# A pooled attention and two feed-forward layers in one kernel: the pooled rows of v are summed by TensorE instead of VectorE and DRAM

## The chip, the cores and the metric

The kernel runs on one core of one Trainium2 chip. The metric is device time in microseconds (us) of one execution, the median of several. Engines are named as the profile names them: PE is TensorE, DVE is VectorE, ACT is ScalarE, POOL is GpSimd, SP is SyncE, whose queue (SPq) issues nearly all transfers here.

## The reference

Attention over q, k, v of shape 4 batches x 8 heads x 576 positions x 64, in two parts that are added, followed by two feed-forward layers over 2304 tokens of width 512.

```python
q_d = q.reshape(B, H, Sd, factor, D).mean(axis=3)    # factor 4, Sd 144
k_d = k.reshape(B, H, Sd, factor, D).mean(axis=3)
v_d = v.reshape(B, H, Sd, factor, D).mean(axis=3)
out_d = sm_attn(q_d, k_d, v_d)                       # coarse: 144 x 144 a head
out_up = np.repeat(out_d, factor, axis=2)
mask = np.abs(pos[:, None] - pos[None, :]) < factor  # local: a band of 7
scores = np.where(mask, scale * q @ k.T, -1e9)
out_local = softmax(scores) @ v
x = out_up + out_local
# then rms norm, silu(x @ w_gate) * (x @ w_val) @ w_out, and relu(h)^2 layer
```

## The kernel before

**Coarse heads.** There are 32 of them (4 batches of 8), and PE takes them in 35 *slots*, `for n in range(HEADS + VAL_LAG)`. Slot n holds, in this order: 1 dummy matmul (3 in slots up to 8) that does nothing but keep PE running (L1845); the scores of head n (L1882); dummies again; the transposes of the exponentials of head n-2 (L1894); the value products of head n-3 (L1916); and, if `slot_units(n)` names one, a *unit*: the transposes that bring a third of one batch's pooled q or k into place (`turn_pooled`, L1864). Slots 5 to 10 hold the units of batch 1, slots 12 to 17 those of batch 2, slots 20 to 25 those of batch 3. For each head DVE takes the least score (`least`, L1567), ACT makes the exponentials (L1263) and copies the transposes out (`keep_turned`, L1255), and after each unit ACT copies it out of its PSUM bank CTR (`keep_pooled`).

**Rows of v for the coarse heads.** The four neighbouring rows of v have to be added. For batch 0 the rows come in two halves (`rawv0`, 72 partitions), and DVE adds them (`pool_v0`, L1544 and L1545) straight to `dv`, from which PE reads. For batches 1 to 3 `pool_v` (L1010, L1013) adds them on DVE in a layout of 128 partitions, ACT's queue stores the sum to DRAM (`store_vd`), and SP's queue loads it back in the layout of 72 partitions (`load_dv`). SP's queue is in order: `load_dv(1)` waits for that store, and all loads written behind it wait as well.

**Local part.** Tokens are cut into five tiles of 128 groups. POOL multiplies q and k windows (`qk_mult(a, n)`, 16 products a tile, L551) and probabilities and v windows (`pv_mult`, L565); DVE adds each product up (`qk_reduce` L596, `pv_reduce` L606); two product buffers tie the two together: product i waits until product i-2 was added up. Tile 0 holds its v windows in four places, so that heads 4 to 7 load only when a place comes free.

**Feed-forward.** After slot 34 PE runs 66 steps of gate, value and out matmuls (L782, L816 to L818): 18 for tile 0 (twelve of 256 columns, six of 512), then 12 for each further tile. Each weight piece is loaded, split in a high part (ACT, `weight_hi`) and a low part (`weight_lo`, mostly DVE). Tile 1's steps need tile 1's attention, made by POOL and DVE meanwhile. The order on each engine is written out by hand; DVE's has `hidden_mul(0)`, which waits for the first gate and value matmuls, ahead of `qk_reduce(1, 4)`. The second layer follows (L904 to L906, L922 to L924).

Of the kernel before, what the change touches and what calls it, by code (L numbers as in the profile page):

```python
# [44 lines left out]
UNIT0 = [("q", 0), ("k", 0), ("q", 1), ("k", 1), ("q", 2), ("k", 2)]  # L45
UNIT = [("q", 0), ("q", 1), ("k", 0), ("k", 1), ("q", 2), ("k", 2)]
UNITS = len(UNIT)
HEADS = B * H
# [7 lines left out]
UNIT_FROM = {1: 5, 2: 4, 3: 4}  # L56
# [14 lines left out]
PRODUCTS = [("qk", 0, n) for n in range(16)] + [("pv", 0, n) for n in range(16) if n not in ACT_PV[0]] + [("qk", 1, n) for n in range(16)]  # L71
# [75 lines left out]
def slot_units(n):  # L147

    for b in range(1, B):
        i = n - H * (b - 1) - UNIT_FROM[b]  # L150
        if 0 <= i < UNITS:
            return ((b, i),)
    return ()


def build(nc, q, k, v, w_gate, w_val, w_out, rms_g, w2_in, w2_out, s2, b2, out):
    y_scr = nc.dram_tensor("y_scr", [TILES, P, DT, W_], F32, kind="Internal").ap()
    c_scr = nc.dram_tensor("c_scr", [G, E], F32, kind="Internal").ap()
    v_scr = nc.dram_tensor("v_scr", [B, H * J, D], F32, kind="Internal").ap()

    with ExitStack() as ctx:
# [79 lines left out]
        rawv = [None] + [place(at, f"rawv{b}", [P, QT, FAC * D], F32) for b in (1, 3)]  # L241
        vs2 = place(at, "vs2", [P, 2, WIN * D], F32)
        assert at[0] <= att_start
        at = [wo_start]
        cs = place(at, "cs", [P, 4, 2 * J], F32)
# [5 lines left out]
        rawv = [None, rawv[1], place(at, "rawv2", [P, QT, FAC * D], F32), rawv[2]]  # L251
# [3 lines left out]
        kd = place(at, "kd", [P, 2, QT, D], F32)  # L255
        qd = place(at, "qd", [P, QT, D], F32)
        vd = place(at, "vd", [P, QT, D], F32)
# [47 lines left out]
        q0_pooled, k0_pooled, v0_pooled = sem("q0_pooled"), sem("k0_pooled"), sem("v0_pooled")  # L305
        rawv_loaded = [sem(f"rawv_loaded{b}") for b in range(B)]
        vd_stored, dv_loaded = sem("vd_stored"), [sem("dv_loaded0"), sem("dv_loaded1")]
        k_order, q_pooled = sem("k_order"), sem("q_pooled")
        k_pooled = [sem(f"k_pooled{b}") for b in range(B)]
        v_half, v_pooled = [sem(f"v_half{b}") for b in range(B)], [sem(f"v_pooled{b}") for b in range(B)]  # L310
# [9 lines left out]
        v_loaded = [sem(f"v_loaded{i}") for i in range(WSLOTS0)]  # L320
# [83 lines left out]
        def weight_hi(act, n):  # L404
# [5 lines left out]
            if n == FIRST_ORDER.index(("out", 0)):  # L410
                act.wait_ge(cpv, HEADS)
            if n >= NW1:
# [22 lines left out]
        def load_piece(sp, n):  # L435
            src, hi, lo, rows = piece(n)
            wait(sp, w_lo[n % SLOTS], n // SLOTS)
            if n == 0:
                sp.wait_ge(prod_ready, qk_at(0, 15) + 1)
# [55 lines left out]

        def q_win(a, h):
            n = slot_of(a, h)
            return qs[:, n, :] if n < 2 else qs2[:, n - 2, :]
# [5 lines left out]
        def v_win(a, h):  # L504
            n = slot_of(a, h)
            return vs[:, n, :] if n < 2 else vs2[:, n - 2, :]
# [13 lines left out]
        def load_v(sp, a, h):  # L520
            last = before_in_slot(a, h)
# [6 lines left out]
            load_window(sp, v, v_win(a, h), a, h, v_loaded[slot_of(a, h)], 48)  # L528
# [24 lines left out]
        def pv_mult(pool, a, n):  # L553
# [4 lines left out]
            if half == 0 or by_act(a, n - 1):  # L558
                pool.wait_ge(v_loaded[slot_of(a, h)], 48 * slot_turn(a, h))
# [7 lines left out]
        def pv_taps(act, a, n, f):  # L567

            h, half = divmod(n, 2)
            if f == 0:  # L570
                act.wait_ge(probs, a + 1)
                act.wait_ge(v_loaded[slot_of(a, h)], 48 * slot_turn(a, h))
# [413 lines left out]
        def store_vd(eng, b):  # L986
            eng.wait_ge(v_pooled[b], 1)
            eng.dma_start(v_scr[b].rearrange("(p t) d -> p t d", p=P), vd[:, :, :]).then_inc(vd_stored, 16)
# [990 lines left out]
```

## Time and profile before

| what | value |
|---|---|
| median of 3 runs | 980.24 us (979.86 to 981.27) |
| the profiled execution, its own time | 984.85 us |
| its span | 982.9 us |
| PE busy | 949.1 us, 97% |
| DVE busy | 537.4 us, 55% |
| ACT busy | 354.0 us, 36% |
| POOL busy | 368.4 us, 37% |

The profiled execution is 4.6 us above the median, and its span leaves out 1.95 us that lie around it. Engines overlap, so their busy times don't add up to the span. PE's busy time holds dummies, and it holds slow stretches too, in which PE was granted half of its clock; the windows below have the granted clock in their own column.

### The profile page before, as it was taken

The page shows a single profiled execution, that of the slowest core. Times are in us where ns is not written, and L with a number is a line of the kernel's source. Part 1 is how long each engine was busy: PE and PEld are TensorE (multiplying, and loading weights), DVE is VectorE, ACT ScalarE, POOL GpSimd, SP SyncE. Part 2 cuts the span into 40 slices and gives each one's busy share as a digit, 9 for nine tenths or more (in the row PEclk, how much of TensorE's full clock was granted, in tenths as well). Part 3 has the DMA queues.
Part 4 walks back from the last instruction along what each step waited for, and adds up shares of the span by engine and source line. Part 5 has one row for each costly group of instructions (what it writes and reads, how often), then busy time and mean ns, then how long its engine had stood idle before and what let it go on. Part 6 is the DMA issues. An engine that isn't in the chain of part 4 may idle for free.

```text
span 982.9 us, 13208 instructions
## 1 busy us (share of the span) xinstructions
PE 949.1 (97%) x5008; PEld 766.3 (78%) x5031; DVE 537.4 (55%) x813; ACT 354.0 (36%) x816; POOL 368.4 (37%) x192
## 2 busy tenths in 40 slices
PE   7888899989999999999999999999999999999998
PEld 4677699756777777777778998888888888888897
DVE  6888997886775765564542224444433443343343
ACT  2448854752324232422241444222322322222232
POOL 4757866777783876465600454000000000000000
PEclk9898799999999999999999999999999999999999
DMA  9898673433331331012003341102001100100010
GB/s 244 217 259 253 180 216 94 147 87 104 97 111 35 86 106 48 15 38 70 19 9 120 130 129 64 43 1 86 1 1 43 43 0 1 65 1 1 1 43 22
DMA packets 54379, 79.42 MB, mean 81 GB/s; under 512 B 9836, under 2 KB 37068, under 8 KB 52908
## 3 DMA queue, kind: packets, MB, share of 16 engines
q1 hardware_dynamic: 52284, 71.53, 24.8%
q10 hardware_dynamic: 2032, 7.05, 1.9%
q8 instruction: 40, 0.66, 0.3%
q14 instruction: 23, 0.19, 0.1%
HBM read 67.05 MB, written 11.50 MB: 80 GB/s over the span
## 4 chain that ended last, share of the span: by engine, by line
PE 78%; DVE 6%; DMA 4%; POOL 3%; ACT 3%; issue 2%; SPq 2%; ACTq 0%; DVEq 0%; POOLq 0%
PE bank L782 23%; PE bank L922 7%; PE bank L923 7%; PE bank L924 7%; PE bank L905 7%; PE bank L906 7%; PE bank L904 7%; PE bank L818 4%; PE bank L816 4%; PE bank L817 4%; POOL prod L551 3%; DMA rawv<-in_v_dram 2%; ACT prod_a L578 1%; DMA vs<-in_v_dram 1%; PE bank L726 1%
## 5 line engine op out<-in xcount | busy, mean ns | idle before, releaser
L551 POOL TENSOR_TENSOR prod<-qs,ks 128x896 f32<-128x896 f32 x80 | 177.7, 2244 | 89.7 <-DVE sc L596 62.9
L565 POOL TENSOR_TENSOR prod<-sc,vs 128x896 f32<-128x896 f32 x72 | 136.7, 2001 | 64.8 <-DVE x L606 32.7
L945 DVE SCALAR_TENSOR_TENSOR r<-bank,r 128x512 f32<-128x512 f32 (+1 forms) x80 | 51.1, 638 | 181.0 <-ACT r L933 181.0
L906 PE MATMUL bank<-y_h,w2i_l 128*128 128x512 f32 (+1 forms) x320 | 117.7, 368 | 0.0
L933 ACT ACTIVATE r<-bank 128x512 f32<-128x512 f32 (+1 forms) x80 | 44.4, 555 | 181.9 <-PE bank L906 181.2
L838 DVE TENSOR_TENSOR bank<-bank,u 128x512 f32<-128x512 f32 (+1 forms) x66 | 39.6, 599 | 118.0 <-PE bank L782 113.0
L782 PE MATMUL bank<-x_h,wv_h 128*128 128x512 f32 (+1 forms) x264 | 100.0, 390 | 0.0
L596 DVE TENSOR_REDUCE sc<-prod 128x14 f32<-128x896 f32 x80 | 85.7, 1078 | 18.0 <-POOL prod L551 18.0
L816 PE MATMUL bank<-h_h,wo_h 128*128 128x512 f32 (+1 forms) x264 | 93.1, 353 | 0.0
L818 PE MATMUL bank<-h_h,wo_l 128*128 128x512 f32 (+1 forms) x264 | 92.6, 351 | 0.0
L817 PE MATMUL bank<-h_l,wo_h 128*128 128x512 f32 (+1 forms) x264 | 92.5, 351 | 0.0
L782 PE MATMUL bank<-x_h,wg_h 128*128 128x512 f32 (+1 forms) x264 | 89.1, 359 | 1.0 <-ACT u L826 0.9
L782 PE MATMUL bank<-x_l,wv_h 128*128 128x512 f32 (+1 forms) x264 | 90.1, 353 | 0.0
L782 PE MATMUL bank<-x_l,wg_h 128*128 128x512 f32 (+1 forms) x264 | 88.2, 356 | 0.3 <-DVE x_l L759 0.3
L606 DVE TENSOR_REDUCE x<-prod 128x128 f32<-128x896 f32 x72 | 77.6, 1080 | 14.7 <-POOL prod L565 14.1
L922 PE MATMUL bank<-w2o_ha,g_h 128*128 128x512 f32 x216 | 84.3, 390 | 0.4 <-ACT y_st L852 0.4
L923 PE MATMUL bank<-w2o_la,g_h 128*128 128x512 f32 x216 | 84.2, 390 | 0.0
L924 PE MATMUL bank<-w2o_ha,g_l 128*128 128x512 f32 x216 | 84.0, 389 | 0.0
L939 ACT ACTIVATE g_h<-r 128x512 fp32r<-128x512 f32 (+1 forms) x80 | 47.1, 589 | 101.1 <-DVE r L947 101.1
L826 ACT ACTIVATE u<-bank 128x512 f32<-128x512 f32 (+1 forms) x66 | 34.2, 518 | 128.6 <-PE bank L782 128.5
L953 DVE TENSOR_TENSOR g_l<-r,g_h 128x512 fp32r<-128x512 f32 (+1 forms) x80 | 51.2, 639 | 52.5 <-ACT g_h L939 52.5
L832 ACT ACTIVATE h_h<-bank 128x512 fp32r<-128x512 f32 (+1 forms) x66 | 34.3, 519 | 110.1 <-DVE bank L838 110.1
(142 smaller groups left out, 1935.7 us busy)
## 6 DMA issues: line engine op xcount, KB each, us to landing
raww<-in_moe_w_out_dram SPq DMA_DIRECT2D x14, 512.0 KB, 4.1
ks<-in_k_dram SPq DMA_DIRECT2D x16, 280.0 KB
vs<-in_v_dram SPq DMA_DIRECT2D x16, 280.0 KB, 5.0
y_scr<-y_st ACTq DMA_DIRECT2D x4, 1024.0 KB, 5.7
raww<-in_moe_w_in_dram SPq DMA_DIRECT2D x8, 512.0 KB, 3.5
y_raw<-y_scr SPq DMA_DIRECT2D x4, 1024.0 KB, 4.8
out_dram<-o_st SPq DMA_DIRECT2D x16, 256.0 KB, 2.8
rawq<-in_q_dram SPq DMA_DIRECT2D x3, 1152.0 KB, 15.2
```

The source lines that it names most:

```text
L551: pool.tensor_tensor(dst, qv, kv, ALU.mult).then_inc(prod_ready, 1)
L565: pool.tensor_tensor(dst, pv, vv, ALU.mult).then_inc(prod_ready, 1)
L596: dve.tensor_reduce(sc[:, a % 2, n * 2 * BAND:(n + 1) * 2 * BAND], prod[:, at_ % 2, :].rearrange("p (s d) -> p s d", d=D), op=ALU.add, axi ...
L606: dve.tensor_reduce(x[:, 2 * half:2 * half + 2, h * D:(h + 1) * D], over(prod[:, at_ % 2, :], [[BAND * D, 2], [BAND, D], [1, BAND]]), op=A ...
L782: last = pe.matmul(o[:, 0:w], wt[:, m, kk, :], xs[:, kk, cols], start=i == 0, stop=i == 3 * DT - 1)
L816: pe.matmul(o, wo_h[:, m, cols], h_h[:, s % 3, 0:w], start=m == 0 and p != 1, stop=False)
L817: pe.matmul(o, wo_h[:, m, cols], h_l[:, s % 3, 0:w], start=False, stop=False)
L818: last = pe.matmul(o, wo_l[:, m, cols], h_h[:, s % 3, 0:w], start=False, stop=m == M1 - 1)
L906: last = pe.matmul(o, w2i_l[:, m, kk, :], y_h[t % 2][:, kk, 0:w], start=False, stop=kk == DT - 1)
L922: pe.matmul(o, g_h[:, r % 3, cols], wh[:, mh, :], start=m == 0, stop=False)
L923: pe.matmul(o, g_h[:, r % 3, cols], wl[:, mh, :], start=False, stop=False)
L924: last = pe.matmul(o, g_l[:, r % 3, cols], wh[:, mh, :], start=False, stop=m == M2 - 1)
```

## The change

The four rows of v are added by PE: four matmuls whose stationary operand is the identity, 72x72, and whose moving operand is rows of v, 72x512, in float32, accumulate in the bank CTR; ACT copies the result to `dv`. These are two more units a batch, ("v", 0) and ("v", 1). `pool_v0`, `pool_v`, `store_vd`, `load_dv` and the DRAM scratch go. Rows of v of all batches load in halves of 72 partitions, and each later half waits until PE has read the half before it in its buffer. Units now stand in slots 2 and 3 (the two v units of batch 0), 4 to 11, 12 to 19 and 20 to 27. Tile 0 gets eight places for v windows. The first two products of tile 1 move ahead of tile 0's pv products on POOL, `weight_lo(1)` moves behind `least(30)` on DVE.

```diff
-UNIT = [("q", 0), ("q", 1), ("k", 0), ("k", 1), ("q", 2), ("k", 2)]
+UNIT = [("q", 0), ("q", 1), ("k", 0), ("k", 1), ("v", 0), ("q", 2), ("k", 2), ("v", 1)]
+QK0 = 6
-UNIT_FROM = {1: 5, 2: 4, 3: 4}
+UNIT_FROM = 4
...
+    if n in (2, 3):
+        return ((0, QK0 + n - 2),)
+    b, i = divmod(n - UNIT_FROM, UNITS)
+    return ((b + 1, i),) if 0 <= b < B - 1 else ()
...
             if n < SLOTS:
-                eng.wait_ge(v_pooled[1], 1)
-                eng.wait_ge(v_pooled[3], 1)
+                eng.wait_ge(ctr_ps, UNITS * B)
...
-        def load_dv(eng, b):
-            eng.wait_ge(vd_stored, 16 * b)
-            wait(eng, cpv, H * (b - 1))
-            eng.dma_start(dv[0:JH, b % 2, :, :], v_scr[b].rearrange("(n p) d -> p n d", p=JH)).then_inc(dv_loaded[b % 2], 16)
...
-            load_rawv0(0)
+            load_rawv(0, 0)
+            load_qk(sp, 0, 1)
             load_rawq(1)
-            load_qk(sp, 0, 1)
+            load_rawv(0, 1)
             load_qk(sp, 0, 2)
-            load_rawv0(1)
...
+                if b > 1:
+                    sp.wait_ge(ctr_ps, UNITS * (b - 1) + UNIT.index(("v", g)) + 1)
+                sp.dma_start(rawv[1 + g][0:JH, :, :], rows).then_inc(rawv_loaded[g], 16)
...
+                if kind == "v":
+                    wait(act, cpv, H * (b - 1))
+                    act.activation(dv[0:JH, b % 2, H * g:H * (g + 1), :], CTR[0:JH, :].rearrange("p (h d) -> p h d", d=D), ACT.Copy).then_inc(ctr_evac, 1)
...
+                if kind == "v":
+                    if b == 0:
+                        pe.wait_ge(rawv0_loaded[g], 16)
+                    else:
+                        pe.wait_ge(rawv_loaded[g], 16 * b)
+                    pe.wait_ge(ctr_evac, n)
+                    rows = rawv0[0:JH, H * g:H * (g + 1), :] if b == 0 else rawv[1 + g][0:JH, :, :]
+                    for f in range(FAC):
+                        last = pe.matmul(CTR[0:JH, :], ident[0:JH, 0:JH], rows[:, :, f * D:(f + 1) * D], start=f == 0, stop=f == FAC - 1)
```

On PE, slots 2 to 4 of the kernel before, from the transposes of head 0 on (L1845 dummies, L1882 scores, L1894 transposes, L1916 value products, L1864 a unit of q):

```order
L1894 MATMUL bank<-ident,cs 72x72 x4
L1845 MATMUL bank<-ident 128x512 x3
L1882 MATMUL bank<-kT,qT 72x144 x2
L1845 MATMUL bank<-ident 128x512 x3
L1894 MATMUL bank<-ident,cs 72x72 x4
L1916 MATMUL bank<-dv,cpT 72x64 x4
L1845 MATMUL bank<-ident 128x512 x3
L1882 MATMUL bank<-kT,qT 72x144 x2
L1845 MATMUL bank<-ident 128x512 x3
L1894 MATMUL bank<-ident,cs 72x72 x4
L1916 MATMUL bank<-dv,cpT 72x64 x4
```

The same place of the changed kernel (its line numbers are its own: L1836 dummies, L1884 scores, L1896 transposes, L1917 value products, L1852 the new v units):

```order
L1896 MATMUL bank<-ident,cs 72x72 x4
L1852 MATMUL bank<-rawv_104,ident 72x512 x4
L1836 MATMUL bank<-ident 128x512 x3
L1884 MATMUL bank<-kT,qT 72x144 x2
L1836 MATMUL bank<-ident 128x512 x3
L1896 MATMUL bank<-ident,cs 72x72 x4
L1917 MATMUL bank<-dv,cpT 72x64 x4
L1852 MATMUL bank<-rawv_104,ident 72x512 x4
L1836 MATMUL bank<-ident 128x512 x3
L1884 MATMUL bank<-kT,qT 72x144 x2
L1836 MATMUL bank<-ident 128x512 x3
```

The scores of head 4 now stand behind both v units of batch 0, the second of which waits for the second half of batch 0's rows (`rawv0_loaded1`).

On SP's queue, the loads behind the last q and k windows of tile 0, before (L1036 rows of v of batch 2, L475 v windows, L1025 rows of q of batch 3, L994 `load_dv(2)`):

```order
L1036 DMA rawv_103<-in_v_dram 128x2304
L475 DMA vs<-in_v_dram 16x448
L475 DMA vs<-in_v_dram 15x192
L475 DMA vs<-in_v_dram 112x640
...
L1025 DMA rawq_106<-in_q_dram 128x9x256
L994 DMA dv<-v_scr 72x16x64
```

and in the changed kernel (L1030 the two halves of batch 2, L474 v windows, L528 the q window of tile 1's head 0):

```order
L1030 DMA rawv_94<-in_v_dram 72x8x256
L1030 DMA rawv_95<-in_v_dram 72x8x256
L474 DMA vs<-in_v_dram 16x448
L474 DMA vs<-in_v_dram 15x192
L474 DMA vs<-in_v_dram 112x640
...
L528 DMA qs<-in_q_dram 16x256
```

The wait for a store to DRAM has gone from the queue; in its stead the two halves wait for PE's units in slots 8 and 11, and all loads behind them with them.

## Rows read from the trace of the kernel before

**Rows 1.** Windows by stage: us, then busy us (x instructions), granted PE clock, DMA share, GB/s

```profile
13.50:38.80 25.30, 20.16 (x158) 14.33 (x155) 17.96 (x22) 9.98 (x42) 14.31 (x7) 1.00 1.06 242
38.80:71.80 33.00, 28.56 (x237) 24.03 (x237) 27.20 (x36) 13.65 (x54) 20.10 (x10) 0.86 0.88 247
71.80:122.70 50.90, 43.49 (x331) 36.66 (x329) 47.42 (x80) 43.15 (x160) 40.12 (x19) 0.77 0.70 208
122.70:209.00 86.30, 86.09 (x582) 74.92 (x585) 74.53 (x89) 51.63 (x129) 62.27 (x29) 0.97 0.51 150
209.00:231.00 22.00, 17.05 (x71) 11.27 (x71) 14.38 (x33) 10.24 (x17) 12.67 (x6) 0.92 0.22 63
231.00:983.00 752.00, 745.48 (x3601) 601.00 (x3620) 346.51 (x545) 221.84 (x408) 211.06 (x103) 1.00 0.15 49
```

**Rows 2.** Timeline of PE, slot 13: start, us, what

```profile
55.44 0.38 PE L1845 MATMUL bank<-ident 128*128 128x512 bf16 x1
55.65 0.66 PE L1882 MATMUL bank<-kT,qT 72*72 72x144 f32 x4
56.14 0.38 PE L1845 MATMUL bank<-ident 128*128 128x512 bf16 x1
56.36 0.41 PE L1894 MATMUL bank<-ident,cs 72*72 72x72 f32 x4
56.61 0.68 PE L1916 MATMUL bank<-dv,cpT 72*72 72x64 f32 x8
57.13 0.82 PE L1864 MATMUL bank<-ident,rawq 128*64 128x128 f32 x6
57.78 0.38 PE L1845 MATMUL bank<-ident 128*128 128x512 bf16 x1
```

**Rows 3.** Timeline of PE: where slots 4, 8 and 18 begin

```profile
20.52 0.81 PE L1845 MATMUL bank<-ident 128*128 128x512 bf16 x3
...
38.11 0.89 PE L1845 MATMUL bank<-ident 128*128 128x512 bf16 x3
...
71.38 0.63 PE L1845 MATMUL bank<-ident 128*128 128x512 bf16 x1
```

**Rows 4.** Timeline of PE: first transposes of x, first gate matmuls

```profile
115.38 1.94 PE L726 MATMUL bank<-ident,x 128*128 128x128 f32 x8 [1.38 <-ACT x L707]
...
122.69 1.20 PE L782 MATMUL bank<-x_h,wg_h 128*128 128x256 f32 x4
```

**Rows 5.** Instructions on rawv: duration ns min/median/max, first and last start

```profile
L1010 DVE TENSOR_TENSOR rawv<-rawv x3: 1343/1360/2649, 41.5 to 92.1; 128x1152 f32<-128x1152 f32 x3
L1013 DVE TENSOR_TENSOR vd<-rawv x3: 757/2141/2619, 42.9 to 93.5; 128x576 f32<-128x576 f32 x3
...
L1544 DVE TENSOR_TENSOR rawv<-rawv x2: 1211/2174/3137, 17.9 to 30.5; 72x1024 f32<-72x1024 f32 x2
L1545 DVE TENSOR_TENSOR dv<-rawv x2: 687/688/689, 19.1 to 33.7; 72x512 f32<-72x512 f32 x2
```

**Rows 6.** Waits of SP's queue to 125 us: us in total, times, longest

```profile
SPq L994 <- DMA v_scr<-vd: 34.8, 3, 15.5
```

**Rows 7.** Timeline of DVE: the second half of batch 0's v arrives

```profile
30.52 3.14 DVE L1544 TENSOR_TENSOR rawv<-rawv 72x1024 f32<-72x1024 f32 x1 [0.53 <-DMA rawv<-in_v_dram]
```

**Rows 8.** The page's groups of instructions: busy us, mean ns | idle before

```profile
L596 DVE TENSOR_REDUCE sc<-prod 128x14 f32<-128x896 f32 x80 | 85.7, 1078 | 18.0 <-POOL prod L551 18.0
...
L832 ACT ACTIVATE h_h<-bank 128x512 fp32r<-128x512 f32 (+1 forms) x66 | 34.3, 519 | 110.1 <-DVE bank L838 110.1
```

**Rows 9.** Windows after PE had sat idle: columns as in rows 1

```profile
37.40:44.00 6.60, 6.57 (x35) 4.90 (x36) 4.82 (x5) 1.61 (x6) 5.15 (x3) 0.60 1.02 244
...
68.90:82.80 13.90, 13.51 (x75) 11.15 (x76) 12.26 (x22) 9.72 (x42) 7.96 (x4) 0.52 0.70 207
...
110.00:127.00 17.00, 15.43 (x92) 13.68 (x93) 16.49 (x36) 13.53 (x33) 12.40 (x5) 0.51 0.45 135
```

**Rows 10.** Timeline of POOL: products of tile 1 after the first gate matmuls

```profile
130.51 11.31 POOL L551 TENSOR_TENSOR prod<-qs,ks 128x896 f32<-128x896 f32 x4 [5.64 <-DVE sc L596]
```

More of the change, by code:

```diff
@@ L69 @@
 ACT_PV = {0: (2, 6, 10, 13), 1: (2, 6, 10, 13)}
-PRODUCTS = [("qk", 0, n) for n in range(16)] + [("pv", 0, n) for n in range(16) if n not in ACT_PV[0]] + [("qk", 1, n) for n in range(16)]
+PRODUCTS = [("qk", 0, n) for n in range(16)] + [("qk", 1, 0), ("qk", 1, 1)]
+PRODUCTS += [("pv", 0, n) for n in range(16) if n not in ACT_PV[0]] + [("qk", 1, n) for n in range(2, 16)]
 EARLY = {2: 2, 3: 4, 4: 4}
@@ L240, in build @@
         at = [gl_start]
-        rawv = [None] + [place(at, f"rawv{b}", [P, QT, FAC * D], F32) for b in (1, 3)]
+        rawv = [None] + [place(at, f"rawv{g}", [P, H, FAC * D], F32) for g in range(2)]
+        at = [gl_start + 2 * QT * FAC * D * 4]
         vs2 = place(at, "vs2", [P, 2, WIN * D], F32)
@@ L244, in build @@
         at = [wo_start]
+        vs3 = place(at, "vs3", [P, H - WSLOTS0, WIN * D], F32)
         cs = place(at, "cs", [P, 4, 2 * J], F32)
@@ L319, in build @@
         qk_loaded = [sem(f"qk_loaded{i}") for i in range(WSLOTS0)]
-        v_loaded = [sem(f"v_loaded{i}") for i in range(WSLOTS0)]
+        v_loaded = [sem(f"v_loaded{h}") for h in range(H)]
         prod_ready, prod_used = sem("prod_ready"), sem("prod_used")
@@ L494, in before_in_slot, with v_turn, v_before @@
             return (0, h + WSLOTS0) if a == 1 else (a - 1, h + H - 2)
+        def v_turn(a, h):
+            return 1 if a == 0 else 1 + (H // 2) * (a - 1) + h // 2 + 1
+        def v_before(a, h):
+            if a == 0:
+                return None
+            if h >= 2:
+                return (a, h - 2)
+            return (0, h) if a == 1 else (a - 1, h + H - 2)
         def q_win(a, h):
@@ L504, in v_win @@
         def v_win(a, h):
-            n = slot_of(a, h)
-            return vs[:, n, :] if n < 2 else vs2[:, n - 2, :]
+            n = h if a == 0 else h % 2
+            return vs[:, n, :] if n < 2 else vs2[:, n - 2, :] if n < WSLOTS0 else vs3[:, n - WSLOTS0, :]
         def load_qk(sp, a, h):
@@ L520, in load_v @@
         def load_v(sp, a, h):
-            last = before_in_slot(a, h)
+            last = v_before(a, h)
             if last is not None:
@@ L1144, in _ @@
             pool.memset(ident[:, :], 0.0).then_inc(consts_made, 1)
-            for s_ in (ks, vs, ks2, vs2):
+            for s_ in (ks, vs, ks2, vs2, vs3):
                 last = pool.memset(s_[0:1, :, 0:(FAC - 1) * D], 0.0)
@@ L1265, in exponents @@
                                    accum_out=csum[0:JH, b % 2, 2 * h + a, 0:1]).then_inc(cexp, 1)
-            for i in range(UNITS):
+            for i in range(QK0):
                 keep_pooled(0, i)
@@ L1615, in _ @@
             least(15)
-            pool_v(dve, 2)
             least(16)
@@ L1622, in _ @@
             least(17)
+            qk_reduce(dve, 1, 0)
             softmax_norm(dve, 0)
+            qk_reduce(dve, 1, 1)
             pool_q(3)
@@ L1660, in _ @@
             add_pooled0(dve, 1)
-            weight_lo(dve, 1)
             least(29)
@@ L1664, in _ @@
             least(30)
-            qk_reduce(dve, 1, 0)
+            weight_lo(dve, 1)
             exponent_sums(3, 0)
@@ L1668, in _ @@
             least(31)
-            qk_reduce(dve, 1, 1)
             exponent_sums(3, 1)
@@ L1865, in turn_pooled @@
                     else:
-                        last = pe.transpose(to, qd[:, 3 * g + t, :] if kind == "q" else kd[:, 0, 3 * g + t, :], ident[:, :])
+                        last = pe.transpose(to, qd[:, 3 * g + t, :] if kind == "q" else kd[:, 3 * g + t, :], ident[:, :])
                 last.then_inc(ctr_ps, 1)
-            for i in range(UNITS):
+            for i in range(QK0):
                 turn_pooled(0, i)
                 if i % 2:
-                    keep_running(CSC[0], 3 if i < UNITS - 1 else 2)
+                    keep_running(CSC[0], 3 if i < QK0 - 1 else 2)
             for n in range(HEADS + VAL_LAG):
@@ L1905, in _ @@
                     pe.wait_ge(cpt_evac, g + 1)
[L1906 to L1909 removed]
+                    if h % 4 == 0:
+                        pe.wait_ge(ctr_evac, UNITS * b + (UNIT if b else UNIT0).index(("v", h // 4)) + 1)
+                    if h == 0:
                         wait(pe, co_ready, 2 * b - 1)
```

133 lines of the change are left out of this document (55 added, 78 removed).

## The prediction

> **What bounds the kernel now.** I read the windows by stage first [rows 1]. From 231 us on PE is busy 745.5 of 752 us at full clock: nothing in the change touches this part, so the kernel ends when it does because of the time at which this part begins. From 122.7 to 209 us PE is busy 86.1 of 86.3 us, with the steps of tile 0. Between them, 209 to 231 us, PE sits idle for 5.0 us and is granted 0.92 of its clock: it waits there for tile 1's attention. So two things can move the end: the time at which the coarse heads let PE go (122.69 us, the first gate matmul [rows 4]), and the time at which tile 1 is ready.
>
> The change works in the stretch before 122.7 us. There, from 13.5 us on, PE is busy 92.2 of 109.2 us, DVE 92.6, ACT 66.8, POOL 74.5 (the sums of the first three of rows 1). No engine is full; DVE and PE are nearest, and PE lost about as much by its clock (granted 0.86 and 0.77 in the second and third, 4.6 + 11.7 us) as it sat idle (17.0 us). SP's queue stood 34.8 us behind the trips through DRAM [rows 6].
>
> How full PE really is, one slot tells [rows 2]. Slot 13, with one dummy at a time and a unit of q, begins at 55.44 us and the next at 57.78: 2.34 us with no gap in it. Its parts, from start to start: a dummy 0.21, scores 0.49, a dummy 0.22, transposes 0.25, value products 0.52, the unit 0.65.
>
> **What goes.** On DVE ten additions: L1010 5.35 us in all, L1013 5.52, L1544 4.35, L1545 1.37 [rows 5], together 16.6 us. ACT loses three issues of stores. SP's queue loses the 34.8 us, but not for free, see below.
>
> **What comes on PE.** The trace has no float32 matmul of 512 columns that isn't rounded. The nearest row is the scores: two matmuls of 144 columns appear as four records and take 0.49 us [rows 2], 0.85 ns a column and record. At two records a matmul, 512 columns take 0.87 us, a unit of four 3.48 us, and the eight units 27.9 us at full clock, twice that at half. Bound below: one record a column, 13.9 us; above, the value products (eight records of 64 columns in 0.52 us, 1.02 ns) give 33 us. I take 27.9, because the scores are the same kind of instruction with the longer moving operand. A slot with a v unit then takes 2.34 - 0.65 + 3.48 = 5.17 us, one with no unit 1.69.
>
> The Trainium skill, in TensorE: Matmul & The Clock Gate, section Back-to-back issue gap, gives N / 2.4 GHz plus 2.5 ns a matmul, 0.216 us for 512 columns, and that would make 6.9 us of the eight units instead of 27.9. The trace disagrees for this type: by that rule two scores would take 0.13 us, and they take 0.49 [rows 2].
>
> **On ACT** eight copies of 72x512. The nearest row is `hidden_hi`, 519 ns [rows 8]: 4.2 us. ACT is busy 66.8 of 109.2 us and each copy stands behind the exponentials of its slot, so I cost it at nothing; if ACT is the one that holds a slot up (slots 19 to 27, where it also makes products of tile 0), it costs up to 0.5 us each, 1.6 us for the three units there. The new memset of vs3 and the loads of tile 0's last v windows are hidden: their products come tens of us later.
>
> **Slot by slot.** Before, slot 4 begins at 20.52 us [rows 3]. The first v unit puts 3.5 us ahead of that: 24.0. The second half of batch 0's rows arrived at 30.5 us [rows 7], which only DVE had to wait for, and PE worked on with slots 4 to 6. Now PE itself waits for it at the end of slot 3, with every later slot queued behind, and DVE, ACT and POOL behind PE's scores. One set of q and k windows (408 KB) fewer stands ahead of it: 1.7 us at 242 GB/s [rows 1]. So it lands at 28.8 us, PE sits idle 4.8 us, and slot 4 begins at 28.8 + 3.5 = 32.3.
>
> Slots 4 to 7 have six dummies each: 2.34 + 4 x 0.22 = 3.22 us, 12.9 together. Pooled k of batch 1 is made by DVE behind `least(6)` and a reduction (1.08 us [rows 8]), then 1.34 us of its own (same shape as L1010 [rows 5]); the reduction and the addition, 2.4 us, run while PE does 1 us of slot 6: I add 1.4. Slot 8 begins at 46.6, where it began at 38.11 [rows 3]: 8.5 us late.
>
> The clock: after an idle stretch PE was granted 0.60 for 6.6 us, or 0.52 for 13.9 us [rows 9], which lost 2.6 or 6.7 us. The new idle of 4.8 us will do one of the two; nothing excludes that it costs none. I take 2.6, the nearer in place, so slot 8 begins 11.1 us late.
>
> Slots 8 to 17 at full clock: slot 8 has six dummies and a v unit, 6.05; slots 11 and 16 5.17 each; the other seven 2.34 each; 32.8 us. Before they took 71.38 - 38.11 = 33.3 us [rows 3], with idle and slow stretches. So slot 18 begins 10.6 us late, and the unit time is paid for by idle time that PE had anyway.
>
> Slots 18 to 30 and the part of slot 31 ahead of x's transposes: three slots with v (19, 24, 27), seven with q or k (18, 20 to 23, 25, 26), three empty, and 1.2 us: 15.5 + 16.4 + 5.1 + 1.2 = 38.2 us. Before it was 115.38 - 71.38 = 44.0 us [rows 3, 4], a good part of it at 0.52 of the clock [rows 9] and behind ACT and DVE. With DVE 3.5 us lighter here and PE fuller, I take 2 us of idle: 40.2, so 3.8 us are given back. The transposes of x start 6.8 us late. DVE's chain for tile 0 does not come earlier: its last reduction stands behind `least(28)`, and that behind PE's slot 28.
>
> From the transposes to the first gate 7.3 us [rows 4], kept. The gate starts 6.8 us late.
>
> **After the gate.** POOL waits 5.64 us for `qk_reduce(1, 4)` [rows 10]. In DVE's order this stands behind `hidden_mul(0)`, and that behind PE's first value matmuls. So tile 1's chain moves with PE's gate; that POOL has two of tile 1's products behind it already only lengthens this wait. `weight_lo(1)`, moved behind `least(30)`, holds back piece 5 on SP's queue and two windows of tile 1 behind it, to about the time of that wait: nothing more. The idle time at 209 us stays as it is, since both its sides moved alike. For small slack on DVE I take off 0.3 us.
>
> **The sum.** 3.5 (first unit) + 4.8 (wait) + 3.5 (second unit) + the longer slots 4 to 7, so that slot 8 is 8.5 late; + 2.6 (clock) - 0.5 - 3.8 - 0.3 = +6.5 us. Against the profiled execution: its span goes from 982.9 to 989.4 us, its own time from 984.85 to 991.4. That execution lies 4.6 us above the median, so the median goes from 980.24 to 986.7 us.
>
> The skill also has a rule that speaks for the change: SBUF — State Buffer, section SBUF: two separate sides, says that a DVE operation with two SBUF inputs and a GpSimd operation lock each other out of a shared port pair. The trace agrees: the same addition took 757 and 2619 ns [rows 5]. By it POOL gains too, at most the 16.6 us of these additions, but POOL's products stand behind DVE's reductions and those behind PE's scores.
>
> **The rivals.**
> *DVE's relief and the free queue win (faster).* For it: DVE busy 47.4 of 50.9 us, and 34.8 us of SP's wait. The point from which it decides: the second half of v lands by 24.0 us and PE never drops its clock. Then slot 8 is 3.7 late, slot 18 3.2, the transposes 3.2 + 38.2 - 44.0 = 2.6 early, and the stretch of 17 us at 0.51 [rows 9] runs at full clock, of which I count 2.4 more. 980.2 - 5 = 975.2. Against it: loads were full all the while (DMA share 1.06 [rows 1]).
> *The delay is swallowed (no change).* PE has 5.0 us idle at 209 to 231 us and slow clock there [rows 1]: about 6.5 us. If tile 1 did not depend on the gate, that would hold 6.5 us of delay: 980.2. Against it stands the order on DVE.
> *PE stays at half clock (much slower).* A second drop like that of 13.9 us, 6.7 us [rows 9]: 993.4.
> *The units are cheap.* By the row of bf16 dummies (0.21 us for 512 columns [rows 2]) the eight cost 6.9 us. The wait for the second half stays, but slot 8 is then 5.9 late, slots 8 to 17 take 25.0 us and 18 to 31 30.4: whatever else binds then is DVE, with 16.6 us less; 976.
> The skill's rule on the issue gap, above, is this last rival.
> That the change doesn't do what it says, also partly holds: SP's queue trades the wait for DRAM for waits on PE's slots 8, 11, 16 and 19. That is in the forecast, since windows still arrive in time.
>
> **How the numbers follow.** Forecast 0.56, relief wins 0.17, swallowed 0.12, half clock 0.12, cheap units 0.03. The forecast's own bounds: clock cost 0 instead of 2.6, idle in slots 18 to 31 0 instead of 2, 982; clock cost 6.7 and idle 5, 994. The range 979 to 994.5 leaves out most of the two faster rivals, and little above. Within 0.2% (about 2 us, what a measurement of this kernel can tell from no change): the swallowed case and the lower edge of the forecast, 0.14. Faster 0.19, slower 0.67.
>
> **What the profile would show.** PE idle for some 5 us before the second v unit, its wait being a transfer; v units of 3.5 us at full clock; slot 18 at about 82 us; x's transposes at about 122; a lower granted clock behind the wait; POOL's wait ahead of the products of tile 1's head 3 longer than 5.64 us; DVE some 16 us lighter. I am wrong if the half lands much earlier, if PE's clock holds up and the transposes come by 115, or if the gap at 209 us shrinks with a late gate.

## The result, and the profile after

The changed kernel takes 1006.0 us (median of 4, 1002.91 to 1008.01) against 980.75 of the kernel before on the same chip: ratio 1.025, interval 1.0217 to 1.0284. It is slower, as forecast, but the forecast was 986.7 and its range ended at 994.5.

The windows of the profiled execution after (span 1003.7 us), columns as in [rows 1] (the window and its length; then busy us and instructions of PE, of PE's weight loads, of DVE, ACT and POOL; then the granted clock, the DMA share and GB/s):

```profile
13.50:38.80 25.30, 22.43 (x98) 11.35 (x97) 7.97 (x12) 6.88 (x27) 12.04 (x6) 0.80 1.04 234
38.80:81.66 42.86, 41.47 (x329) 30.04 (x328) 27.51 (x40) 20.63 (x75) 27.12 (x13) 1.00 0.78 202
81.66:138.30 56.64, 50.25 (x313) 34.92 (x311) 36.15 (x64) 38.92 (x146) 30.95 (x15) 0.79 0.44 115
```
```profile
144.34:230.64 86.30, 83.97 (x585) 72.86 (x584) 76.07 (x90) 51.99 (x130) 67.50 (x30) 1.00 0.53 156
230.64:252.64 22.00, 17.28 (x73) 11.70 (x72) 14.47 (x33) 10.22 (x17) 12.70 (x6) 0.92 0.23 64
```

The second fence is the two windows that answer to 122.7 to 209 and 209 to 231 us of [rows 1], counted from the first gate matmul. They are the old ones, moved by 21.65 us: the first gate matmul begins at 144.34 us and not at 122.69 [rows 4], the span grows by 20.8. So everything was lost before the gate. The first fence cuts that part at slot 18 (81.66 us) and at x's transposes (138.30 us). Up to slot 18 things stand where the forecast had them. Slots 18 to 31 take 56.6 us, where it had 40.2 and where they took 44.0.

TensorE in slots 3 and 19 (timeline: start, us, what, [idle before it <- what ended it]; L1852 is the v unit, L1917 a value product):

```profile
22.42 0.68 PE L1917 MATMUL bank<-dv,cpT 72*72 72x64 f32 x8
25.97 7.06 PE L1852 MATMUL bank<-rawv,ident 72*72 72x512 f32 x8 [2.87 <-DMA rawv<-in_v_dram]
32.82 1.06 PE L1836 MATMUL bank<-ident 128*128 128x512 bf16 x2
```
```profile
87.62 1.20 PE L1917 MATMUL bank<-dv,cpT 72*72 72x64 f32 x8 [2.27 <-DVE co L1554]
89.82 7.07 PE L1852 MATMUL bank<-rawv,ident 72*72 72x512 f32 x8 [1.00 <-ACT kT L1247]
96.68 0.63 PE L1836 MATMUL bank<-ident 128*128 128x512 bf16 x1
```

A v unit at full clock takes 3.44 us from start to start (75.87 to 79.31 in slot 16). Both of these stand behind waits (2.87 us; 2.27 and 1.00 us), run at half clock, and take 6.85. The second wait was not in the forecast: VectorE's `finish_pooled(1, 0)` (L1554) frees the bank that the value product needs. Before, the pair of which it is the first ran on VectorE from 75.13 us for 1.28 us, the value product came at 76.92, and nobody waited. The window from 87.6 to 108.0 us shows what followed, a granted clock of 0.50 for 20.4 us:

```profile
87.60:108.00 20.40, 19.38 (x74) 12.24 (x75) 10.88 (x15) 9.26 (x38) 9.55 (x6) 0.50 0.69 169
```

VectorE just ahead of it (L607 reduces a tile's score products, L635 to L646 are the softmax of tile 0, L1534 pools q):

```profile
78.00 1.00 DVE L635 SCALAR_TENSOR_TENSOR sc<-sc,mask 128x224 f32<-128x224 f32 x1
79.04 0.39 DVE L637 TENSOR_REDUCE smax<-sc 128x32 f32<-128x224 f32 x1
79.46 1.73 DVE L638 TENSOR_TENSOR sc<-sc,smax 128x224 f32<-128x224 f32 x1
81.11 0.44 DVE L1563 TENSOR_REDUCE cneg<-bank 72x2 f32<-72x288 f32 x1
81.48 1.07 DVE L607 TENSOR_REDUCE sc<-prod 128x14 f32<-128x896 f32 x1
...
83.48 0.39 DVE L646 TENSOR_TENSOR sc<-sc,ssum 128x224 f32<-128x224 f32 x1
83.79 1.08 DVE L607 TENSOR_REDUCE sc<-prod 128x14 f32<-128x896 f32 x1
84.78 2.09 DVE L1534 TENSOR_TENSOR rawq<-rawq 128x1152 f32<-128x1152 f32 x1
86.80 1.27 DVE L1554 TENSOR_TENSOR co<-bank,rsum 72x512 f32<-72x512 f32 x2
```

GpSimd beside it (L562 multiplies q and k windows, L576 probabilities and v windows):

```profile
76.68 4.26 POOL L562 TENSOR_TENSOR prod<-qs,ks 128x896 f32<-128x896 f32 x2 [1.39 <-DVE sc L607]
83.95 4.59 POOL L576 TENSOR_TENSOR prod<-sc,vs 128x896 f32<-128x896 f32 x2 [3.00 <-DVE sc L646]
```

The same operations in the kernel before (L624, L627 and L1531 are L635, L638 and L1534 of the changed kernel, L1558 is its L1554), and TensorE's value product that needs the last of them:

```profile
70.83 0.39 DVE L624 SCALAR_TENSOR_TENSOR sc<-sc,mask 128x224 f32<-128x224 f32 x1
...
71.68 0.39 DVE L627 TENSOR_TENSOR sc<-sc,smax 128x224 f32<-128x224 f32 x1
...
73.86 1.35 DVE L1531 TENSOR_TENSOR rawq<-rawq 128x1152 f32<-128x1152 f32 x1
75.13 1.28 DVE L1558 TENSOR_TENSOR co<-bank,rsum 72x512 f32<-72x512 f32 x2
```
```profile
76.92 1.15 PE L1916 MATMUL bank<-dv,cpT 72*72 72x64 f32 x8
```

The two L607 at 81.48 and 83.79 are tile 1's, which the change moved here. And while GpSimd makes products, VectorE's operations with two SBUF inputs are slow: L638 takes 1.73 us, where the same operation took 0.39 before, beside an idle GpSimd. In experiment 11, with the products moved back, it takes 0.39 again.

From this I had two theories. W: the loss is TensorE's added work, one for one. C: it is the waits of the new arrangement, and the half clock behind each.

### The profile page after: what moved, and what is told of

Its sections match the earlier page's. It is cut to its first block, busy times and chain, and to the rows that moved or that the text cites. A ratio compares the mean times of both kernels' runs of the same rounds, so it can differ in the third digit from the quotient of the medians.

```text
span 1003.7 us, 13361 instructions
## 1 busy us (share of the span) xinstructions
PE 976.9 (97%) x5095; PEld 771.8 (77%) x5095; DVE 523.4 (52%) x803; ACT 360.0 (36%) x824; POOL 371.4 (37%) x193
## 4 chain that ended last, share of the span: by engine, by line
PE 90%; DVE 3%; DMA 2%; ACT 2%; issue 1%; SPq 1%; POOL 1%; ACTq 0%; DVEq 0%; POOLq 0%
PE bank L793 28%; PE bank L933 7%; PE bank L934 7%; PE bank L935 7%; PE bank L916 6%; PE bank L917 6%; PE bank L915 6%; PE bank L829 5%; PE bank L827 5%; PE bank L828 5%; PE bank L1852 3%; DMA rawv<-in_v_dram 2%; PE bank L1836 1%; PE bank L1884 1%; PE bank L1866 1%
## 5 line engine op out<-in xcount | busy, mean ns | idle before, releaser
L562 POOL TENSOR_TENSOR prod<-qs,ks 128x896 f32<-128x896 f32 x80 | 179.9, 2270 | 101.7 <-DVE sc L607 80.1
L576 POOL TENSOR_TENSOR prod<-sc,vs 128x896 f32<-128x896 f32 x72 | 136.8, 2002 | 66.4 <-DVE x L617 39.9
L607 DVE TENSOR_REDUCE sc<-prod 128x14 f32<-128x896 f32 x80 | 85.5, 1077 | 18.0 <-POOL prod L562 17.8
```

What stands on the lines that cost most here:

```text
L562: pool.tensor_tensor(dst, qv, kv, ALU.mult).then_inc(prod_ready, 1)
L576: pool.tensor_tensor(dst, pv, vv, ALU.mult).then_inc(prod_ready, 1)
L607: dve.tensor_reduce(sc[:, a % 2, n * 2 * BAND:(n + 1) * 2 * BAND], prod[:, at_ % 2, :].rearrange("p (s d) -> p s d", d=D), op=ALU.add, axi ...
```

## The experiments

Each ratio is to the kernel before on the same chip, with its 95% interval; the change itself stands at 1.025.

**1. Less work in the same place.** `rows[:, :, 0:D]` in place of the loop over `f`, so one matmul a unit.

> The changed kernel with one matmul in each of the eight v units, in place of four: only the first of the four rows of v is taken, the other three are left out of the sum. A unit should take about 0.9 us at full clock, not 3.44, so about 20 us of TensorE's work are gone and every wait of the change stays possible. Theory W (TensorE's added work is the loss, one for one, since TensorE is the bound of the stage): 1005 less 20, about 985. Theory C (most of the loss comes from two waits of TensorE, on v's rows in slot 3 and on finish_pooled(1, 0) in slot 19, and from the half clock behind them): the units between the slots go, but the waits stay or grow, about 995; the profile must then still show a wait of over 2 us in slot 19 and half clock behind it. If both count, between 978 and 995.

987.9 us, 1.0075 [1.0046, 1.0103]. By the ratios 17 us came back for 20.6 us of matmuls, nearer to W's 985 than to C's 995. But the waits grew, as C says: TensorE's two long waits are

```profile
29.27 1.13 PE L1851 MATMUL bank<-rawv,ident 72*72 72x512 f32 x1 [7.25 <-DMA rawv<-in_v_dram]
83.19 1.19 PE L1916 MATMUL bank<-dv,cpT 72*72 72x64 f32 x8 [6.10 <-DVE co L1554]
```

The time alone doesn't decide: 6.9 us of added matmuls remain, and the kernel is 7.4 us slower than before. What W has no place for is the 13.35 us of waiting in these two lines. Each is longer than in the changed kernel, so part of the matmuls taken out only turned into waiting.

**2. The late bank, by a direct move.**

```
+            finish_pooled(1, 0)
             softmax_max(dve, 0)
```

> The changed kernel with VectorE's finish_pooled(1, 0) ahead of softmax_max(0) in place of behind softmax_norm(0) and pool_q(3). The result is needed by TensorE's value product of slot 19. Theory C: the 2.27 us wait in slot 19 goes, and with it the half clock over slots 19 to 22 (some 8 to 10 us); 994 to 997. Rival W: the clock falls anyway or the chain waits elsewhere, 1002 to 1006.

1004.3 us, 1.027 [1.022, 1.032]: no gain. VectorE now stood still itself, for the store of batch 0's result, which `finish_pooled(1, 0)` must not overtake:

```profile
79.46 0.69 DVE L1554 TENSOR_TENSOR co<-bank,rsum 72x512 f32<-72x512 f32 x1 [4.09 <-DMA c_scr<-co]
```

The softmax came later by that, ScalarE with it, and TensorE waited 2.12, 1.10 and 2.44 us for ScalarE in slots 18 and 19. The time is the rival's, and the wait moved on as the rival says. Whether the first wait cost anything the run doesn't tell, since it put others in its place.

**3. The late rows.** `if n in (2, 4)` for batch 0's units, `UNIT_FROM = 5`, ScalarE's copies likewise.

> The changed kernel with the second v unit of batch 0 in slot 4, not 3, and all later units one slot later, ScalarE's copies with them. In the changed kernel TensorE waited 2.87 us in slot 3 for the second half of v's rows and ran the unit and the next slot at half clock until 32.8 us. Theory C: the wait goes, and with it 3 us of wait and about 4 us of half clock, if nothing waits later: about 998 to 1000. Rival: the gain is swallowed by the wait in slot 19, which is set by VectorE and GpSimd, not by TensorE: 1003 to 1006.

996.7 us, 1.017 [1.014, 1.020]: 7.5 us back. The wait of slot 3 is gone, slot 18 begins at 73.1 us and not at 81.66. The work is the same, so W alone is refuted. The wait for L1554 stays (2.57 us), and the unit behind it runs at half clock.

**4. No work on TensorE, no trip.** VectorE adds v's halves straight into `dv`:

```
-            pool_v(dve, 1)
+            pool_v(1, 0)
+            pool_v(1, 1)
...
-                        pe.wait_ge(dv_loaded[b % 2], 16 * ((b + 1) // 2))
```

> The kernel before, with the trip through DRAM gone and the additions left on VectorE: v's rows of batches 1 to 3 come in two halves on 72 partitions, as in the changed kernel, and VectorE adds them straight into the places that TensorE reads. TensorE has no v units; no eight places, no moved products. If the loss of the change is TensorE's work and what its order does, none of it is here: 976 to 981. VectorE has some 8 us more work than before in all; if that counts at TensorE's bound, 983 to 986.

986.7 us, 1.007 [1.004, 1.010]: slower than before. There are 16 additions in place of 10 (medians 1.22 and 0.69 us, the longest 2.95), VectorE is busy for 543.1 us and not 537.4, and TensorE waits for ScalarE 3.33, 2.05, 2.31 and 2.37 us. So without the trip through DRAM, 34.8 us of SP's queue [rows 6], nothing is gained if VectorE has more to do for it. What the trip costs alone is not shown: the run takes it away and adds work to VectorE at once.

**5. The products back.**

```
-PRODUCTS = [... for n in range(16)] + [("qk", 1, 0), ("qk", 1, 1)]
-PRODUCTS += [("pv", 0, n) ...] + [("qk", 1, n) for n in range(2, 16)]
+PRODUCTS = [... for n in range(16)] + [("pv", 0, n) ...] + [("qk", 1, n) for n in range(16)]
```

> The changed kernel with the first two products of tile 1 back behind tile 0's value products, on GpSimd, and their two reductions on VectorE back to the end of the coarse heads. In the changed kernel VectorE's softmax of tile 0 ran beside these products (1.00 and 1.73 us for operations that took 0.39 before) and two reductions of 1.07 us stood ahead of finish_pooled(1, 0): some 4.9 us, against TensorE's wait of 2.27 us in slot 19. Theory C: the wait goes and so does the half clock over slots 19 to 22; 995 to 999. Rival W (the work is the loss, the clock falls anyway): 1003 to 1006.

1002.8 us, 1.019 [1.013, 1.026]. The profiled execution is the odd one of four: 990.9 us, the others 1002.0 to 1003.7. In it the rows of slot 3 came in time,

```profile
23.63 3.65 PE L1851 MATMUL bank<-rawv,ident 72*72 72x512 f32 x8 [0.50 <-DMA rawv<-in_v_dram]
```

a wait of 0.50 us and not 2.87, the unit at full clock, slot 4 at 27.1 us and not at 32.8. The others left no trace; that they waited as the changed kernel does would explain part of the 12 us, but is only argued. Their times are the rival's (1003 to 1006) and not C's (995 to 999). The wait for L1554 is gone. In its place the v unit of slot 19 waits 1.98 us for ScalarE, and the clock falls: the unit takes 5.0 us. So C's form, in which the wait for `finish_pooled(1, 0)` itself is the loss, fails here.

**6. Both of these.** Edits 3 and 5 together.

> The last one and the later second half (its v unit in slot 4, all later units one slot later, 996.6 us alone) together. Theory C: both long waits of TensorE are gone and the clock stays full up to slot 24; 988 to 992, the eight v units' own time less what before lost at half clock. Rival: the two edits mend the same loss and give no more than the late half alone: 995 to 998.

992.6 us, 1.012 [1.006, 1.018], just above C's 988 to 992. The four executions lie from 988.2 to 999.5 us, and the interval takes in the 1.017 of experiment 3 alone, so the rival is not excluded.

**7. The work alone, on the kernel before.**

```
+                if n in (2, 3, 8, 11, 16, 19, 24, 27):
+                    for _ in range(4):
+                        pe.matmul(CSC[(n + 1) % 3][0:JH, :], ident[0:JH, 0:JH], over(ident[0:JH, 0:], [[0, 4], [1, P]]), ...)
```

> The kernel before with TensorE's added work alone: four f32 matmuls of 72 rows and 512 columns, of ones and zeros, at the ends of slots 2, 3, 8, 11, 16, 19, 24 and 27 (the slots of the v units), their sums never read; nothing is taken off VectorE, GpSimd or the queues, and nothing is moved. The work is 27.5 us at full clock. Before, TensorE idled for 17 us between 13.5 and 122.7 us and was at half clock for part of it. If the loss of the change is this work alone: 998 to 1006, as the changed kernel. If the order and the late data make it: the idle time takes some of the work up, 985 to 993.

990.8 us, 1.010 [1.006, 1.013]: 27.5 us of matmuls cost some 9.4 (6 to 13). Up to slot 18 idle time and half clock of [rows 1] took the work up: in the profiled execution, 986.4 us long and the fastest of six, TensorE is hardly idle and has its full clock there:

```profile
13.50:38.00 24.50, 24.43 (x162) 15.18 (x160) 15.50 (x21) 8.80 (x37) 13.14 (x7) 1.00 1.06 281
38.00:73.50 35.50, 35.18 (x269) 25.26 (x270) 29.87 (x41) 16.34 (x63) 22.84 (x9) 1.00 0.71 205
```

**8. The relief alone.** The kernel before without `pool_v(1..3)`, `store_vd` and `load_dv`.

> The kernel before without VectorE's additions for v of batches 1 to 3 and without the trip through DRAM (v's rows are still loaded); the sums of batches 1 to 3 are left out, and the value products of all batches read those of batch 0. It shows what the relief of VectorE and of the queues is worth alone, at most 13 us of VectorE's time. If VectorE sets TensorE's pace between slots 8 and 31: 971 to 976. If not: 978 to 981.

971.8 us, 0.989 [0.983, 0.996]. The relief alone is worth some 10 us (4 to 17). VectorE is busy for 527.2 us and not 537.4. How much of the gain is VectorE's and how much the queue's isn't separated here; after experiment 4, where the queue was freed and VectorE loaded, VectorE's share is the likelier one.

**9. Work and relief, without the arrangement.** Edits 7 and 8 together.

> The kernel before with the relief alone (no additions of v for batches 1 to 3, no trip; these sums are left out) and TensorE's 32 extra matmuls in the slots of the v units: both halves of the trade, and nothing of the order, the data that units wait for, ScalarE's copies or the moved products. If the two add up: 971.8 + 10 = 982, and the other 24 us of the change are its arrangement. If relief and work interact (a lighter VectorE leaves TensorE no idle time to take the work up): 990 to 998.

986.6 us, 1.009 [1.007, 1.011]. They don't add up: 10 us off and 9.4 on would be no change, and it is 8.5 us slower. With TensorE loaded the relief gives nothing that the intervals could tell (1.0096 with the work alone, 1.0087 here). This is what the change is worth as a trade, and it is close to what the forecast gave; the other 16 us are its arrangement. (VectorE still adds batch 0's rows here, which the change also takes off it.)

**10. Batch 0 as before.** VectorE's `pool_v0` for batch 0 again, no units in slots 2 and 3.

> The changed kernel with batch 0's v as before: VectorE adds both halves, at its old places, and TensorE has no v unit in slots 2 and 3; batches 1 to 3 stay changed, the moved products too. Two units (6.9 us at full clock) and the wait for late rows in slot 3 are gone. Theory C (waits and the half clock behind them): the first 9 us of lateness go, but the wait in slot 19 stays; 995 to 999, about as the late half alone (996.6). Theory W (work one for one): 1005 less 7, 998.

998.4 us, 1.020 [1.016, 1.023]: 5 us back, by intervals that overlap. C (995 to 999) and W (998) said the same here. Up to slot 18, which begins at 74.75 us and not at 81.66, not all of the 9 us go: TensorE now waits 2.30 us for VectorE's additions and 2.83 us for batch 1's pooled k, at half clock behind both. The wait in slot 19 stays, as C says: TensorE stands still for L1557, this kernel's `finish_pooled(1, 0)`, for 2.28 us up to 80.7.

**11. And the products back.** Edits 10 and 5 together.

> The last one with tile 1's two products back behind tile 0's value products too. If each of the two arrangements costs time by itself: 986 to 991. If moving the products back gives nothing, as the runs around the profiled one of the back order alone say (1002 to 1004): as the last one.

995.2 us, 1.018 [1.015, 1.020]: the products give 2 us here, within the two intervals, and not the 7 to 12 that were expected if each arrangement costs by itself. VectorE's softmax operations, with GpSimd idle beside them, take 0.39 us again, and the pooling of q, which now begins just ahead of GpSimd's next product (76.07 and 76.24 us), takes 1.35. TensorE's wait for `finish_pooled(1, 0)` is gone, and again another stands in its place:

```profile
78.52 0.68 PE L1921 MATMUL bank<-dv,cpT 72*72 72x64 f32 x8
81.17 7.07 PE L1856 MATMUL bank<-rawv,ident 72*72 72x512 f32 x8 [1.98 <-ACT kT L1244]
88.04 0.63 PE L1840 MATMUL bank<-ident 128*128 128x512 bf16 x1
```

**12. The moved products on the kernel before.**

> The kernel before with the moved products alone: GpSimd multiplies tile 1's first two between tile 0's scores and value products, VectorE reduces them in and behind the softmax of tile 0, and the load for them goes ahead. If the move costs by itself (slower VectorE beside GpSimd and two reductions ahead of finish_pooled(1, 0), which was done 1.2 us before TensorE needed it): 983 to 988. If it is hidden or comes back at the end of the coarse heads, where two products fewer stand: 978 to 981.

983.9 us, 1.004 [1.002, 1.006]. The move costs some 4 us by itself, with no v unit anywhere: VectorE's L625 and L628, the two softmax operations, take 1.13 and 1.74 us, `finish_pooled(1, 0)` ends late, and TensorE stands still longer than in the changed kernel:

```profile
79.28 1.19 PE L1917 MATMUL bank<-dv,cpT 72*72 72x64 f32 x8 [4.62 <-DVE co L1559]
```

**13. ScalarE's copy ahead.** All pooled units of batches 1 to 3 share one bank, so a unit waits until ScalarE has copied the one before it. In slot 19 that copy stood behind both parts of a value product of tile 0 that ScalarE makes (`pv_taps`) and two exponentials. On top of 11:

```
             keep_turned(16)
+            keep_pooled(2, 6)
             pv_taps(act, 0, 2, 1)
             exponents(18)
-            keep_pooled(2, 6)
```

> The changed kernel with batch 0's v on VectorE and tile 1's products back (995.2 us), and ScalarE's copy of the unit of slot 18 ahead of the second of two value products' taps, not behind them and two exponents. The copy should be done at 78.6 and not 80.9 us, before TensorE needs the bank at 79.0. If this stall and the half clock behind it cost the time: slot 20 begins near 83, not 88.5, and the time is 988 to 991. If the clock falls there anyway or the wait moves on: 994 to 997.

989.6 us, 1.009 [1.006, 1.012]. The unit of slot 19 doesn't wait and keeps the full clock:

```profile
75.97 0.68 PE L1921 MATMUL bank<-dv,cpT 72*72 72x64 f32 x8
76.48 3.60 PE L1856 MATMUL bank<-rawv,ident 72*72 72x512 f32 x8
79.93 0.38 PE L1840 MATMUL bank<-ident 128*128 128x512 bf16 x1
```

The scores of slot 20 begin 5.1 us after those of slot 19 (75.0 to 80.2), in 11 it was 10.9. Run again on another chip, beside 14:

> The mended kernel once more: 987 to 992, 0.7 to 1.2% over before.

995.8 us, 1.014 [1.011, 1.017]. The trace shows the same repair (slot 19 at 77.2, slot 20 at 82.3), but the time is above the 987 to 992 expected, and the two intervals only just overlap. So the copy is worth some 4 or 8 us against 11. The traces differ in three places. Up to slot 18 the second is 2.2 us later: VectorE stood still for rows of q (1.13 us, in the first not), and TensorE waited 3.25 us for its pooled k and not 1.39. From slot 18 to x's transposes it takes 48.2 us and not 45.6. The waits there are the same in both, 1.24 and 0.44 us in slot 22, but behind them the clock stays full in the first and falls to half in the second (a dummy takes 0.38 and 0.63 us):

```profile
88.38 0.82 PE L1870 MATMUL bank<-ident,rawk 128*64 128x128 f32 x6 [0.45 <-ACT qT L1244]
89.03 0.38 PE L1840 MATMUL bank<-ident 128*128 128x512 bf16 x1
```
```profile
90.56 1.09 PE L1870 MATMUL bank<-ident,rawk 128*64 128x128 f32 x6 [0.44 <-ACT qT L1244]
91.44 0.63 PE L1840 MATMUL bank<-ident 128*128 128x512 bf16 x1
```

From the first gate matmul to the end the second takes 2.1 us more. So the same waits had the half clock behind them in one execution and not in the other.

**14. Four places for the first tile's v.** `slot_of`, `slot_turn` and `before_in_slot` for v again, on top of 13.

> The mended kernel of before (batch 0's v on VectorE, tile 1's products back, ScalarE's copy ahead) with four places for the first tile's v, as before the change, not eight; the order of the loads stays, so the queue now waits at the fifth head's rows until the first head's products are made. If the eight places carry part of the loss or of the gain by the queue that they keep free: 3 us or more away from the mended kernel. If they only load earlier what is used later: the same within 2 us.

992.3 us, 1.012 [1.009, 1.015], against 1.014 beside it. The medians are 3.5 us apart, the ratios 2, and the intervals overlap: an effect of the eight places is not shown, and one of 2 or 3 us isn't excluded.

**15. and 16. The dummies.** `RUNNING = (3, 0)`, on 13 and on the kernel before.

> The last one without the matmuls that only keep TensorE running, two a slot of 0.22 us each, behind slot 8 (those up to slot 8 stay). If TensorE sets the pace there at full clock, up to 46 of them, 10 us at most, come off: 980 to 986. If they fill time that is then idle and the clock falls with it: no gain, 989 to 1000.

> The kernel before without the same matmuls behind slot 8, as the control. TensorE waited there for others, and the granted clock was 0.77 to 0.86: if the matmuls filled idle time, 979 to 983 with more waits in the profile; if the clock falls further, 985 to 995; if they stood in the way, 972 to 977.

On 13: 999.7 us, 1.020 [1.015, 1.025], 10 us worse than 13. On before: 983.6, 1.004 [1.002, 1.007]. In the first, from slot 18 to slot 31,

```profile
72.50:131.00 58.50, 56.09 (x274) 40.42 (x272) 32.15 (x54) 36.68 (x138) 29.86 (x15) 0.56 0.52 125
```

TensorE is granted 0.56 for 58.5 us. The stretch begins with a wait that 13 doesn't have:

```profile
77.67 0.70 PE L1921 MATMUL bank<-dv,cpT 72*72 72x64 f32 x8 [2.09 <-DVE co L1556]
78.21 5.44 PE L1856 MATMUL bank<-rawv,ident 72*72 72x512 f32 x8
```

VectorE's `finish_pooled(1, 0)` (L1556) was late, because VectorE had itself waited 0.71 us for rows of q and then took 2.29 us to pool them, not 1.35. So leaving the 46 dummies out, 10 us of work at full clock, costs 10 us instead of saving 10. How much of it is the wait, and how much that nothing brought the clock back, one run can't separate. On the kernel before it costs 4. No kernel that computes everything beats the one before.

## Why the prediction was wrong

**What held.** The change's price on TensorE: a unit takes 3.44 us, forecast 3.48. The rule of the Trainium skill (TensorE: Matmul & The Clock Gate, Back-to-back issue gap) gives 0.216 us for 512 columns, so 0.86 for the four, an estimate. The trace agrees with it for the bf16 dummies (0.22 us) and not for these float32 matmuls, which take four times as long. Slot 4 began at 32.8 (forecast 32.3), slot 8 10.8 us late (11.1), slot 18 at 81.66 (82.0). The pooled k of batch 1 held TensorE up for 1.39 us (1.4). The second half's wait and the half clock behind it were there, though split otherwise: 2.87 us idle, not 4.8, and by half clock 3.4 us more for the unit and some 1.7 for slot 4, not 2.6. From the transposes to the gate 6.0 us passed, not 7.3. Behind the gate next to nothing changed, though not by the path that was forecast. GpSimd's wait ahead of the products of tile 1's head 3 should have grown beyond 5.64 us, and it shrank to 0.53; in its place GpSimd waited 8.53 us for windows of head 2, whose load stood behind SP's wait of 34.6 us for piece 5. The end did not feel it. VectorE became 14.0 us lighter (523.4 us busy), not 16. One reading of the rows was off: what the clock took from TensorE's 28.56 and 43.49 busy us is 4.0 + 10.0 us, and the forecast's 4.6 + 11.7 reckons the idle time with it; the sum doesn't use it.

**The step that failed** is "with DVE 3.5 us lighter here and PE fuller, I take 2 us of idle: 40.2". Slots 18 to x's transposes took 56.64 us. Against that sum:

| | forecast | measured |
|---|---|---|
| TensorE busy at full clock | 38.2 | 39.8 (312 matmuls at clock 1.00 in experiment 13; here 313) |
| lost to half clock | 0 | 10.5 (50.25 - 39.76) |
| idle | 2 | 6.4 (56.64 - 50.25) |

16.4 us in all. Together with 0.3 and 1.3 less at the two ends and 0.5 less behind the gate, this makes the span grow by 20.8 us and not by 6.5. The other 5 us of the miss lie outside the kernel's mechanism: the profiled execution of before was 4.6 us above its median, that of after (1005.49) 0.5 below.

Three things stood behind the failed step, and each could be read from the diff and the trace of before. I costed the moved products only at their old place ("that POOL has two of tile 1's products behind it already") and not at the new one; there they put two reductions and slower operations, 4.8 us (two of 1.08, and 0.61, 1.34 and 0.74 more for L635, L638 and L1534 than before), ahead of `finish_pooled(1, 0)`, which had some 1.1 us to spare (done near 75.8 us, wanted at 76.92). I costed ScalarE's copies at nothing, or at most by their length of 0.5 us, and not by the place in its order of the copy *ahead* of each unit, on which the shared bank makes TensorE wait (1.00 us in slot 19 here, 1.98 in 11). And I charged the half clock for one wait, at slot 3, and put it at nothing from slot 18 on, where the waits of 2.27 and 1.00 us had 20.4 us of it behind them.

**The rivals.** *PE stays at half clock* had the right mechanism, but priced one further drop at 6.7 us: there was one of 20.4 us (0.50 from 87.6 to 108.0, 9.7 us of its 19.38 busy us), with waits ahead of it. The half clock near the transposes (0.54 from 135.0 to 142.5) is nothing new: before it was 0.50 from 110.5 to 122.69. *Relief wins* was half true: relief alone gives 10 us (8), but nothing that can be told from noise once TensorE has the work (9). *Swallowed* fell: the gap ahead of tile 1 moved along unchanged. *Cheap units* fell with the unit's 3.44 us. W was refuted by 3 and 7. C in its first form, in which two named waits are the loss, failed in 5 and 11: the wait for `finish_pooled(1, 0)` went, another took its place, and only some 2 to 6 us came back. What is left of C, that the arrangement's waits and the half clock behind them cost time beside the work, is shown by 3, 12 and 13.

**By undoing, in us over the kernel before:** the change 24.5; batch 0's v back on VectorE 19; the products back too 17; ScalarE's copy ahead too 9 to 14; work and relief with none of the arrangement 8.5. Each figure is known to some 3 us, the difference of two to some 4. The forecast's +6.5 lies near that last figure, partly by luck: with no late rows (experiment 9) slot 18 began at 73.1 us and not at 82.0, and slots 18 to 31 took 48.2 and not 40.2, so that too much at one place and too little at another nearly met. The step was too low even without the arrangement.

**Open:** why the clock fell in the repeat of 13 and not in 13, behind the same waits; what the unprofiled executions of 5 did; and what share of experiment 15's loss is its wait.

## What to carry to other kernels

Work moved to an engine with idle time can cost much less than its length (here a third, 9.4 of 27.5 us). But the gain of the relieved engine and this price don't simply add: here the gain of 10 us vanished once the other engine was loaded. The larger loss comes from what goes with the move: for every instruction that moves in any engine's order, look up what stands directly behind its *new* place and how much slack that had; and for a shared buffer, where the release of the *previous* user stands in its engine's order. With a clock that can fall behind a wait, a wait of 2 to 3 us on TensorE can cost more than its length: taking one away gave 7.5 us (3) and 4 or 8 us (13), and nothing where the next wait took its place (2). It need not cost it: behind the wait of 1.39 us at 45.06 in the changed kernel the clock stayed full. And try a schedule in several executions: those of 5 differ by 12 us.

## What was not expected of the hardware

- VectorE's operations with two SBUF inputs took up to 4.5 times as long beside GpSimd's products: 0.39 us became 1.00 and 1.73 (changed kernel), 1.13 and 1.74 (experiment 12); the pooling of q 1.35 became 2.07 to 2.09. Reductions with one input stayed at 1.07. This agrees with the Trainium skill, SBUF — State Buffer, section SBUF: two separate sides, by which a VectorE operation with two SBUF inputs and a GpSimd operation that reads SBUF lock each other out of a shared pair of ports; the forecast used it as a gain only.
- A float32 matmul of 72x512 by a 72x72 identity shows as two records and takes 0.86 us (3.44 for four), 0.84 ns a column and record.
- Behind a wait of 2.27 and one of 1.00 us TensorE was granted 0.50 for 20.4 us, while busy for 19.38 of them; and in 15 it was granted 0.56 over 58.5 us, busy for 56.09. Being busy again did not bring the clock back at once.
- Behind waits of 1.24 and 0.44 us in the same place, the clock stayed full in one execution (13) and fell to half in another (its repeat). So a single trace doesn't tell what a short wait costs.
